# Linear attention feeding two feed-forward stages: where the queries' feature maxima are computed and how they reach the feature map

## The chip, the cores and the metric

The kernel runs on one core of one Trainium2 chip. The metric is device microseconds from the first to the last instruction of a run of the whole program. TensorE (PE in the profile), VectorE (DVE), ScalarE (ACT), GpSimd (POOL) and SyncE (SP, which only issues DMAs here) run side by side and wait for each other through semaphores; each works through its own instructions in program order.

## The reference, cut to what matters

B = H = 8, S = 576 tokens, D = 64, 128 projected features.

```python
def phi(x):                                  # q and k: (8, 8, 576, 64)
    proj = x @ w_phi                         # (..., 576, 128)
    proj = proj - max(abs(proj), axis=-1)    # one maximum per token and head
    return concatenate([exp(proj), exp(-proj)], axis=-1)
q_p, k_p = phi(q), phi(k)
kv  = k_p^T @ v;  z = sum_s k_p
att = (q_p @ kv) / (q_p @ z + 1e-6)          # -> x, (8, 576, 512)
# first feed-forward (phase 1): token shift, xk, xr
y = sigmoid(xr @ w_r) * (relu(xk @ w_k)**2 @ w_v)
# second feed-forward (phase 2)
h = relu(y @ w_in); out = (h * sigmoid(conv3(h))) @ w_out
```

## The kernel before, in words

The program has two phases. Phase 2 (the second feed-forward) isn't touched. Phase 1 does, for each of the 8 batches, the attention of four pairs of heads and the first feed-forward ("MoE" below). It is software-pipelined: one iteration does the MoE of batch m and the attention of batch m+1. `batches` (L338) makes it a prologue (attention of batch 0 alone, with the split of the ten weight pieces in it), an unrolled iteration, a loop of six, and a last iteration with MoE only.

The order of work inside an iteration is written by a planner. `attention_steps` (L48) lists the steps of the four pairs; `iteration` (L81) walks through them with estimated TensorE durations (`PE_NS`, L38) and after a step puts in as many MoE tiles as `FILL_NS` (L41) says, so that TensorE has work while VectorE and ScalarE prepare the next step. The same list of steps drives all engines, so an engine never does a later step's work before an earlier one's. A tile is 12 matmuls of 288 columns in fp32r (each product done in three parts, high and low halves): K tiles (`tile_k`, L558) are drained on ScalarE by relu, square and square again (L678, L681, L683) and one VectorE subtract (L818); R tiles by one tanh (L699); V tiles, two units long, by one VectorE instruction (L825). One iteration has 16 K, 8 R and 16 V units: 480 matmuls.

A pair's steps before the change, with TensorE's instructions (an fp32 matmul shows as two):

- QP: project the queries token by token (tokens on partitions), 10 matmuls of 128 columns, in the two 64-row halves of the array (`project`, L481). VectorE takes the largest magnitude per token from PSUM (L756) and splits it in two fp32r parts (L761, L763).
- KP: the same for the keys, into the same banks, so it waits for L756. VectorE takes the maxima (L767) and subtracts them (L771).
- M: five transposes turn the maxima into rows (L503); ScalarE copies them to SBUF (L644).
- EK: ScalarE makes exp of the shifted keys and of their negative (L649, L651).
- P0, P1: for each half of the tokens, project the queries again with features on partitions (two matmuls of 288 columns) and subtract the maxima by a matmul with a matrix `pick` of -1 rows (two more), all in 64-row halves (`feature_rows`, L507). ScalarE then makes the exponentials (L657).
- KV: sum over tokens, 20 matmuls of 65 columns (`sum_kv`, L522), and a copy (L663).
- DEN, NUM: denominators and numerators (`sum_den` L534, `attend` L548), 8 matmuls of 288 columns each, in 32-column and 64-column quarters and halves of the array; two copies (L668, L673).
- RC, DV: the denominators go to 64 partitions by DMA (L383), VectorE inverts them (L777, L780), they go through DRAM and back (L388, L392), and VectorE divides (L785). Then follow the token shift and its splits (XK/HK/LK and XR/HR/LR, L797, L805, L694, L813).

In PSUM the attention has three banks (ps0) and two (ps1), the MoE three (psm). In the prologue odd pairs use psm instead of ps0, so that a pair's projections can run ahead of the one before.

Of the kernel before, what the change touches and what calls it, by code (L numbers as in the profile page):

```python
# [11 lines left out]
P = 128  # L12
# [6 lines left out]
TT = 5  # L19
# [6 lines left out]
ROWS = D + 2  # L26
# [21 lines left out]
def attention_steps():  # L48

    steps = [("QP", 0)]  # L50
    for p in range(PAIRS):
        steps += [(s, p) for s in ("KP", "M", "EK", "P0", "KV", "P1", "DEN", "NUM")]
        steps += [("QP", p + 1)] if p + 1 < PAIRS else []
    return steps


def first_attention_steps():

    steps = [("QP", 0), ("KP", 0)]
    for p in range(PAIRS):  # L60
        last = p == PAIRS - 1

        def ahead(s):
            return [(s, 0, "next") if last else (s, p + 1)]
# [16 lines left out]
def iteration(with_moe, with_next, ran_ahead=False):  # L81
# [38 lines left out]
    if with_next:  # L120
        fill(FIRST_FILL)
        for step in attention_steps():
            s, p = step[:2]
            if not (ran_ahead and step in (("QP", 0), ("KP", 0))):
                emit(step)
            if with_moe:
                fill(FILL_NS.get(s, 0))
                if s == "DEN":
                    later += [(now + RC_AFTER, ("RC", p)), (now + DV_AFTER, ("DV", p))]
                    later.sort(key=lambda t: t[0])  # L130
                if (s, p) == ("DEN", PAIRS - 1):
                    fill(LAST_FILL)
# [62 lines left out]
def phase_1(nc, ctx, q, k, v, w_phi, mu_k, mu_r, w_k, w_v, w_r, y_scr, den_scr, w_in):  # L195
# [18 lines left out]
    pick = sb_att("pick", [P, F], F32R)  # L214
# [3 lines left out]
    q_max, k_max = sb_att("q_max", [P, 2, TT]), sb_att("k_max", [P, 2, TT])  # L218
    q_max_split = sb_att("q_max_split", [P, TT, 2, D], F32R)
    max_rows = sb_att("max_rows", [P, TT * P], F32R)  # L220
# [3 lines left out]
    pick_f = k_exp[:, 0, 0, :]  # L224
# [19 lines left out]
    ps1 = ctx.enter_context(nc.psum_tensor("ps1", [P, 2 * BANK], F32))  # L244
# [5 lines left out]
    rows_zeroed, tail_zeroed, banks_zeroed, x_zeroed = sem("rows_zeroed"), sem("tail_zeroed"), sem("banks_zeroed"), sem("x_zeroed")  # L250
# [5 lines left out]
    q_projected, k_projected, shared_bank = sem("q_projected"), sem("k_projected"), sem("shared_bank")  # L256
    q_max_ready, q_max_hi, q_max_split_ready = sem("q_max_ready"), sem("q_max_hi"), sem("q_max_split_ready")
    k_max_ready, k_shifted = sem("k_max_ready"), sem("k_shifted")
    max_turned, max_rows_ready = sem("max_turned"), sem("max_rows_ready")
# [3 lines left out]
    den_summed, den_copied = sem("den_summed"), sem("den_copied")  # L263
# [26 lines left out]

    def att_psum(p, a):
        return psm[:].rearrange("p b s -> p (b s)") if first_of(a) and p % 2 == 1 else ps0[:]

    def await_att_psum(eng, p, a):

        if first_of(a):
            await_(eng, den_copied, PAIRS, a, p - 1)
        elif second_of(a) and p == 0:
            eng.wait_ge(den_copied, PAIRS - 1)
        else:  # L300
            await_(eng, den_copied, PAIRS, a, p)
# [19 lines left out]
    def await_bank(eng, t, batch):  # L321
# [3 lines left out]
        if before < 0 and first_of(batch):  # L325
            eng.wait_ge(den_copied, PAIRS)
# [11 lines left out]
    def batches(eng, work):  # L338

        work(None, (None, 0), first_attention_steps())  # L340
        work((None, 0), (None, 1), iteration(True, True, ran_ahead=True))
# [3 lines left out]

    def attention_of(step, a):

        return (None, 1) if step[-1] == "next" else a
# [4 lines left out]
    def _(sp):  # L353

        def load_qk(p, a):

            reg, off = a
            await_(sp, features, H, a, 2 * (p - 1))
# [35 lines left out]
        def work(m, a, steps):  # L394
            if a is not None and not second_of(a):
# [12 lines left out]
            if a is not None and second_of(a):  # L408
                load_qk(1, a)
            pieces = 2  # L410
            for step in steps:
                kind = step[0]
                of = attention_of(step, a)
                if kind == "QP" and step[1] + 1 < PAIRS and step[-1] != "next":
                    load_qk(step[1] + 1, a)
                elif kind == "QP" and step == ("QP", PAIRS - 1) and m is None:
                    load_qk(0, (None, 1))
                if kind == "KV" and step[1] + 1 < PAIRS:
                    load_v(step[1] + 1, a)
                if m is None and kind in ("QP", "KP", "P1") and pieces < len(PIECES):  # L420
# [16 lines left out]
                if kind == "DEN":  # L437
                    spread_den(step[1], of)
                if kind == "RC":
                    repeat_den(step[1], of)  # L440
# [12 lines left out]
    def _(pool):  # L453
        nc.gpsimd.memset(v_nat[:], 0.0).then_inc(zeroed, 1)
        nc.gpsimd.memset(ident[:], 0.0).then_inc(ident_ready, 1)
        nc.gpsimd.memset(pick_f, 0.0).then_inc(pick_made, 1)
# [3 lines left out]
        for n, row in enumerate((0, 1, D, D + 1)):  # L460
            pool.wait_ge(pick_made, 1 + n)
            nc.gpsimd.affine_select(out=pick_f, in_=pick_f, compare_op=ALU.not_equal, fill=-1.0,
                                    base=-row, pattern=[[0, F]], channel_multiplier=1).then_inc(pick_made, 1)
# [693 lines left out]
```

## Time and profile before

| | |
|---|---|
| median of 3 runs | 1418.75 us (1409.08 to 1427.29) |
| the profiled execution | 1417.62 us |
| its span (first to last instruction) | 1415.8 us |
| TensorE busy | 1360.0 us, 96% |
| VectorE, ScalarE busy | 672.6 us (48%), 626.6 us (44%) |
| mean granted TensorE clock | 0.984 of full speed |
| phase 1 ends about | 987 us |

The span is the time from the first to the last instruction of the profiled execution, 1.8 us less than its own time. The busy times of the engines overlap. A matmul's end in the trace is modelled and reaches past the start of the next, so the distance from start to start is what a matmul costs in a stream.

### The profile page before, as it was taken

The numbers are of one execution on the slowest core, as the hardware profiler recorded it, in microseconds if no ns is written. First come the engines' busy times: TensorE is split into PE (matmuls) and PEld (weight loads), VectorE is DVE, ScalarE is ACT, GpSimd is POOL, SyncE is SP. The second block draws the span as 40 slices with busy tenths as digits, with TensorE's granted clock in tenths as the row PEclk, the third lists the DMA queues.
The fourth block names the chain that finished last, engine by engine and source line by source line (L and its number), as shares of the span: only waits on it lengthen the run. The fifth ranks groups of instructions, "written<-read, shape, count | busy, mean of one in ns | idle before, by whom it ended". The sixth has DMA issues, their size and how long they took to land. (4 is left out here: it accounts for less than half of the span.)

```text
span 1415.8 us, 26326 instructions
## 1 busy us (share of the span) xinstructions
PE 1360.0 (96%) x10368; PEld 1211.6 (86%) x10368; DVE 672.6 (48%) x1047; ACT 626.6 (44%) x1111; POOL 13.5 (1%) x18
## 2 busy tenths in 40 slices
PE   5879999999999999999999999998899999999998
PEld 4668899889888889888988888998788988998997
DVE  5444244334433624442544362451757556655753
ACT  3536345454352534545445353443444443433532
POOL 0000000000000000000000000000300000000000
PEclk9879999999999999999999999999999999999999
DMA  5411202202212120220221212030310210110101
GB/s 165 124 45 40 58 27 77 63 20 69 61 45 70 40 58 26 62 78 19 70 54 53 69 41 58 25 116 22 93 64 1 71 64 30 41 63 30 41 30 38
DMA packets 94579, 78.60 MB, mean 56 GB/s; under 512 B 64656, under 2 KB 72976, under 8 KB 93456
## 3 DMA queue, kind: packets, MB, share of 16 engines
q1 hardware_dynamic: 94480, 77.10, 18.2%
q8 instruction: 84, 1.38, 0.4%
q14 instruction: 15, 0.12, 0.0%
HBM read 57.75 MB, written 19.02 MB: 54 GB/s over the span
## 5 line engine op out<-in xcount | busy, mean ns | idle before, releaser
L472 PE MATMUL psm<-xk_hi,wk_hi 128*128 128x288 f32 x512 | 158.6, 310 | 15.1 <-issue 6.9
L969 PE MATMUL psh<-y_hi,win_hi 128*128 128x288 f32 x512 | 153.9, 301 | 13.4 <-ACT h L1054 9.0
L818 DVE TENSOR_TENSOR k_lo<-square,k_hi 128x288 fp32r<-128x288 f32 x128 | 58.7, 458 | 221.3 <-ACT square L683 221.3
L472 PE MATMUL psm<-k_hi,wv_hi 128*128 128x288 f32 x512 | 154.4, 302 | 0.0
L472 PE MATMUL psm<-xk_lo,wk_hi 128*128 128x288 f32 x512 | 153.7, 300 | 0.0
L472 PE MATMUL psm<-xk_hi,wk_lo 128*128 128x288 f32 x512 | 153.2, 299 | 0.0
L970 PE MATMUL psh<-y_lo,win_hi 128*128 128x288 f32 x512 | 152.2, 297 | 0.0
L971 PE MATMUL psh<-y_hi,win_lo 128*128 128x288 f32 x512 | 151.6, 296 | 0.0
L472 PE MATMUL psm<-k_lo,wv_hi 128*128 128x288 f32 x512 | 151.1, 295 | 0.0
L472 PE MATMUL psm<-k_hi,wv_lo 128*128 128x288 f32 x512 | 150.8, 295 | 0.0
L1112 DVE SCALAR_TENSOR_TENSOR conv<-h,taps,conv 128x576 f32<-128x576 f32 x64 | 55.2, 863 | 141.3 <-ACT conv L1056 141.3
L472 PEld LDWEIGHTS psm<-xk_hi,wk_hi 128*128 128x128 f32 x512 | 98.8, 193 | 24.3 <-issue 16.3
L969 PEld LDWEIGHTS psh<-y_hi,win_hi 128*128 128x128 f32 x512 | 97.2, 190 | 16.2 <-ACT h L1054 11.3
L472 PE MATMUL ps<-q_exp,kvz 128*64 128x288 f32 (+1 forms) x992 | 102.1, 409 | 0.5 <-ACT q_exp L657 0.5
L472 PEld LDWEIGHTS psm<-k_hi,wv_hi 128*128 128x128 f32 x512 | 96.3, 188 | 6.6 <-issue 5.8
L678 ACT ACTIVATE relu<-psm 128x288 f32<-128x288 f32 x128 | 51.7, 404 | 113.4 <-PE psm L472 113.4
L971 PE MATMUL pso<-wout_hi,g_lo 128*128 128x512 f32 x256 | 101.1, 395 | 0.0
L969 PE MATMUL pso<-wout_hi,g_hi 128*128 128x512 f32 x256 | 101.0, 395 | 0.0
L970 PE MATMUL pso<-wout_lo,g_hi 128*128 128x512 f32 x256 | 101.0, 394 | 0.0
L1054 ACT ACTIVATE h<-psh 128x576 f32<-128x576 f32 x64 | 41.8, 653 | 129.4 <-DVE gated L1100 94.3
L472 PEld LDWEIGHTS psm<-xk_hi,wk_lo 128*128 128x128 f32 x512 | 98.9, 193 | 0.0
L472 PEld LDWEIGHTS psm<-xk_lo,wk_hi 128*128 128x128 f32 x512 | 98.8, 193 | 0.0
(116 smaller groups left out, 2810.9 us busy)
## 6 DMA issues: line engine op xcount, KB each, us to landing
v_nat<-in_v SPq DMA_DIRECT2D x32, 320.0 KB, 3.6
qk<-in_q SPq DMA_DIRECT2D x32, 288.0 KB, 2.9
qk<-in_k SPq DMA_DIRECT2D x32, 288.0 KB, 3.2
den<-den_scr SPq DMA_DIRECT2D x64, 144.0 KB, 3.0
y_scr<-y SPq DMA_DIRECT2D x64, 144.0 KB, 1.8
y<-y_scr SPq DMA_DIRECT2D x8, 1152.0 KB, 5.5
out<-rows SPq DMA_DIRECT2D x32, 256.0 KB, 2.0
den_parts<-den_rows SPq DMA_DIRECT2D x128, 2.2 KB, 1.9
```

Source lines behind the costliest of these rows:

```text
L472: return nc.tensor.matmul(o, lhsT, rhs, start=first, stop=last)
L678: nc.scalar.activation(relu[:, i % 2, :], psm[:, UNIT["K", n, i] % 3, 0:HALF], ACT.Relu).then_inc(k_relu, 1)
L818: nc.vector.tensor_tensor(k2_lo[:, i, :], square[:, i % 2, :], k2_hi[:, i, :].bitcast(F32), ALU.subtract).then_inc(k2_lo_ready, 1)
L969: nc.tensor.matmul(o, wh, xh, start=first, stop=False, skip_group_check=True)
L970: nc.tensor.matmul(o, wh, xl, start=False, stop=False, skip_group_check=True)
L971: return nc.tensor.matmul(o, wl, xh, start=False, stop=last, skip_group_check=True)
L1054: nc.scalar.activation(two(h[:, j % 2, 1:1 + S]), psh[:, j % 2, :, 0:HALF], ACT.Relu, scale=0.5).then_inc(h_ready, 1)
L1112: nc.vector.scalar_tensor_tensor(out=conv[:, j % 2, :], in0=h[:, j % 2, 0:S], scalar=taps[:, 0, j:j + 1], in1=conv[:, j % 2, :], op0=ALU.m ...
```

## The change

A pair's steps become E, M, KS, PICK, EK, KV, DEN, NUM:

- E (`features_and_keys`): one projection of the queries, features on partitions, left raw in ps0 (four matmuls of 512, 512, 64 and 64 columns), and the ten key tiles of 128 columns, eight into ps1 and two into ps0; all in 64-row halves. It waits for the numerators' copy of the pair before, and three times for matmuls of its own.
- VectorE, `part_maxima`: two transposes in blocks of 32 x 32 of the raw features (576 columns each, from PSUM), maxima and subtract for the last key tile of each head, a reduce of the 1152 turned columns to 36, a copy.
- M: one 128-column transpose. VectorE, `spread_maxima`: a reduce of 128 columns, the split in two parts (32 columns each), and a multiply by a 0/1 mask that spreads the maxima into 18 blocks of 32 columns.
- KS (`shift_keys`): maxima and subtract for the other eight key tiles (1024 columns each).
- PICK (`subtract_maxima`): four matmuls with `pick`, now on all 128 rows, 512 and 64 columns for each head, added onto the raw features. ScalarE makes four exponentials of 576 columns.
- DEN and NUM have the same columns, cut in 64 and 512 instead of twice 288. Both copies follow NUM.
- The copy L644, four of the five transposes, the ten token-by-token query projections, and the prologue's second PSUM home for the next batch's first pair (QP and KP "next") are gone.

The core of the diff:

```diff
-PE_NS = {"QP": 1100, "KP": 1100, "M": 550, "P0": 800, "P1": 800, "KV": 2240, "DEN": 1000, "NUM": 1950,
+PE_NS = {"E": 2800, "M": 150, "PICK": 700, "KV": 4500, "DEN": 1200, "NUM": 2200,
-FILL_NS = {"QP": 2200, "M": 1600, "P0": 3500, "P1": 2600}
-FIRST_FILL, LAST_FILL, RC_AFTER, DV_AFTER = 6000, 1600, 3500, 9000
+FILL_NS = {"E": 3200, "M": 1600, "PICK": 4800, "KV": 1600, "NUM": 1600}
+FIRST_FILL, RC_AFTER, DV_AFTER = 3000, 3800, 9500
...
-    steps = [("QP", 0)]
-        steps += [(s, p) for s in ("KP", "M", "EK", "P0", "KV", "P1", "DEN", "NUM")]
-        steps += [("QP", p + 1)] if p + 1 < PAIRS else []
+    return [(s, p) for p in range(PAIRS) for s in ("E", "M", "KS", "PICK", "EK", "KV", "DEN", "NUM")]
...
-        steps += [("M", p)] + before("RC") + [("P0", p), ("EK", p)] + ahead("QP")
-        steps += [("KV", p), ("P1", p)] + before("DV") + ahead("KP") + [("DEN", p), ("NUM", p)]
+        steps += [("M", p), ("KS", p)] + before("RC") + [("EK", p), ("PICK", p), ("KV", p)] + before("DV")
+        steps += [] if last else [("E", p + 1)]
+        steps += [("DEN", p), ("NUM", p)]
...
+        def features_and_keys(p, a):
...
+            key_tile(0, TT - 1).then_inc(shared_bank, 1)
+            feature_chunk(1, 1, True)
+            feature_chunk(0, 0, True)
+            await_(pe, shared_bank, 3 * PAIRS, a, 3 * p + 1)
+            key_tile(1, TT - 1).then_inc(shared_bank, 1)
+            key_tile(0, 0)
+            key_tile(1, 0)
+            await_(pe, shared_bank, 3 * PAIRS, a, 3 * p + 2)
+            feature_chunk(0, 1, True).then_inc(shared_bank, 1)
+            key_tile(1, 1)
+            key_tile(0, 1)
+            await_(pe, shared_bank, 3 * PAIRS, a, 3 * p + 3)
+            feature_chunk(1, 0, False).then_inc(raw_features, 1)
+            for t in range(2, TT - 1):
+                for h in range(2):
+                    last = key_tile(h, t)
...
+        def part_maxima(p, a):
+            await_(dve, raw_features, PAIRS, a, p + 1)
+            for h in range(2):
+                nc.vector.transpose(q_turn[:, h, :], q_cols(h, p, a)).then_inc(q_turned, 1)
+            nc.vector.tensor_reduce(k_max[:, :, TT - 1], k_tail(p, a), AX.X, ALU.max, apply_absolute_value=True).then_inc(k_tail_max, 1)
...
+            nc.vector.tensor_reduce(q_part[:].rearrange("p (h c) -> p h c", h=4)[:, 0:2, 0:TOK],
+                                    q_turn[:].rearrange("p h (j f) -> p h j f", f=32), AX.X, ALU.max,
+                                    apply_absolute_value=True).then_inc(q_part_once, 1)
...
+        def spread_maxima(p, a):
+            await_(dve, max_turned, PAIRS, a, p + 1)
...
+            nc.vector.tensor_tensor(max_blocks[:], own_block[:].unsqueeze(2).to_broadcast([P, TOK, 32]),
+                                    q_max_split[:].bitcast(F32).unsqueeze(1).to_broadcast([P, TOK, 32]), ALU.mult).then_inc(blocks_ready, 1)
```

The planner's fills give, for one iteration, this order around the waits of the changed steps (K+ is a short third part of a K tile, V- the first half of a V tile): E0, K+ x3, K3, M0, K4, KS0, PICK0, K5, K6, K7, EK0, KV0; E1, R2, RC0, R3, XR, M1, V-0, KS1, PICK1, V0, V-1, V1, EK1, KV1; E2, V-3, RC1, V3, M2, K0, K1, KS2, PICK2, K2, K3, K4, EK2, KV2; E3, K7, RC2, R0, M3, R1, KS3, PICK3, R2, R3, V-0, EK3, KV3.

## Rows read from the trace of the kernel before

**Rows 1.** the page: TensorE's busy time, and its granted clock in 40 slices
```profile
PE 1360.0 (96%) x10368; PEld 1211.6 (86%) x10368; DVE 672.6 (48%) x1047; ACT 626.6 (44%) x1111; POOL 13.5 (1%) x18
...
PEclk9879999999999999999999999999999999999999
```

**Rows 2.** busy time in one loop iteration; columns PE, PEld, DVE, ACT, POOL, clock, DMA
```profile
332.40:450.00 117.60, 116.55 (x996) 102.99 (x996) 49.62 (x84) 54.83 (x104) 0.00 (x0) 1.00 0.19 53
```

**Rows 3.** timeline of TensorE: start us, length, engine, line; steps of one pair
```profile
293.25 1.39 PE L472 MATMUL ps<-phi,qk 64*128 64x128 f32 x20
...
294.57 0.74 PE L503 MATMUL ps<-ident,q_max_split 128*66 128x128 f32 x5
...
295.06 0.38 PE L472 MATMUL psm<-xk_hi,wk_hi 128*128 128x288 f32 x1
...
302.51 2.34 PE L472 MATMUL ps<-v_nat,k_exp 128*128 128x65 f32 x20
...
307.01 0.76 PE L472 MATMUL ps<-qk,phi 64*128 64x288 f32 x4
...
307.83 0.40 PE L472 MATMUL psm<-xr_hi,wr_hi 128*128 128x288 f32 x1
...
309.61 1.15 PE L472 MATMUL ps<-q_exp,kvz 128*1 128x288 f32 x16
...
310.69 0.40 PE L472 MATMUL psm<-xr_hi,wr_hi 128*128 128x288 f32 x1
...
312.48 2.16 PE L472 MATMUL ps<-q_exp,kvz 128*64 128x288 f32 x16
```

**Rows 4.** timeline of TensorE inside a tile of the MoE half
```profile
300.26 0.30 PE L472 MATMUL psm<-xk_lo,wk_hi 128*128 128x288 f32 x1
300.39 0.29 PE L472 MATMUL psm<-xk_hi,wk_lo 128*128 128x288 f32 x1
```

**Rows 5.** timeline of ScalarE at the same place
```profile
301.85 0.41 ACT L678 ACTIVATE relu<-psm 128x288 f32<-128x288 f32 x1
...
302.98 0.39 ACT L678 ACTIVATE relu<-psm 128x288 f32<-128x288 f32 x1
...
304.08 0.39 ACT L678 ACTIVATE relu<-psm 128x288 f32<-128x288 f32 x1
...
304.85 0.43 ACT L683 ACTIVATE square<-relu 128x288 f32<-128x288 f32 x1
```

**Rows 6.** costliest groups, ScalarE and VectorE: busy us, mean ns of one | idle before
```profile
L657 ACT ACTIVATE q_exp<-ps 128x576 f32<-128x576 f32 x128 | 75.6, 642 | 17.5 <-PE ps L472 17.5
...
L805 DVE SCALAR_TENSOR_TENSOR mix<-diff,mu,x 128x288 f32<-128x288 f32 x128 | 60.0, 511 | 2.8
...
L771 DVE TENSOR_TENSOR k_shift<-ps,k_max 128x1280 f32<-128x1280 f32 x30 | 44.7, 1491 | 1.0
...
L767 DVE TENSOR_REDUCE k_max<-ps 128x10 f32<-128x1280 f32 x30 | 44.2, 1475 | 18.1 <-PE ps L472 18.1
...
L649 ACT ACTIVATE k_exp<-k_shift 128x1280 f32<-128x1280 f32 x32 | 40.7, 1271 | 12.9 <-DVE k_shift L771 12.6
...
L785 DVE TENSOR_TENSOR x<-num,den 128x576 f32<-128x576 f32 x32 | 24.1, 754 | 7.0 <-DMA den<-den_scr 7.0
```

**Rows 7.** timeline of SyncE's queue and VectorE, a denominator's round trip
```profile
311.59 2.39 SPq L383 DMA_DIRECT2D den_parts<-den_rows  x4
...
315.36 0.17 DVE L777 SCALAR_TENSOR_TENSOR den_cols<-den_parts 128x9 f32<-128x9 f32 x1 [9.59 <-DMA den_parts<-den_rows]
...
317.24 1.11 SPq L392 DMA_DIRECT2D den<-den_scr  x2
```

**Rows 8.** timeline of TensorE at the end of a loop iteration
```profile
451.05 0.37 PE L472 MATMUL psm<-xk_hi,wk_hi 128*128 128x288 f32 x1 [2.10 <-issue]
```

**Rows 9.** busy time shortly after it, columns as in rows 2
```profile
452.00:455.30 3.30, 3.30 (x16) 3.30 (x15) 0.00 (x0) 0.00 (x0) 0.00 (x0) 0.50 0.80 249
```

**Rows 10.** timeline of TensorE, first matmul of the MoE half
```profile
94.37 0.58 PE L472 MATMUL psm<-xk_hi,wk_hi 128*128 128x288 f32 x1 [4.46 <-DVE xk_lo L813]
```

More of the change, by code:

```diff
@@ L123, in iteration @@
             s, p = step[:2]
-            if not (ran_ahead and step in (("QP", 0), ("KP", 0))):
-                emit(step)
+            emit(step)
             if with_moe:
                 fill(FILL_NS.get(s, 0))
-                if s == "DEN":
+                if s == "NUM":
                     later += [(now + RC_AFTER, ("RC", p)), (now + DV_AFTER, ("DV", p))]
                     later.sort(key=lambda t: t[0])
-                if (s, p) == ("DEN", PAIRS - 1):
-                    fill(LAST_FILL)
         if with_moe:
@@ L394, in work @@
         def work(m, a, steps):
-            if a is not None and not second_of(a):
+            if a is not None:
                 load_qk(0, a)
@@ L436, in work @@
                         sp.dma_start(early.y[:], y_scr[0]).then_inc(early.y_loaded, 16)
-                if kind == "DEN":
-                    spread_den(step[1], of)
+                if kind == "NUM":
+                    spread_den(step[1], a)
                 if kind == "RC":
-                    repeat_den(step[1], of)
+                    repeat_den(step[1], a)
                 if kind == "V":
@@ L459, in _ @@
                                 pattern=[[-1, P]], channel_multiplier=1).then_inc(ident_ready, 1)
[L460 to L463, printed above, removed]
+        nc.gpsimd.memset(own_block[:], 0.0).then_inc(own_made, 1)
+        for q in range(4):
+            pool.wait_ge(own_made, 1 + q)
+            nc.gpsimd.affine_select(out=own_block[:], in_=own_block[:], compare_op=ALU.not_equal, fill=1.0, base=-32 * q,
+                                    pattern=[[-1, TOK]], channel_multiplier=1).then_inc(own_made, 1)
         pool.wait_ge(zeroed, 1)
@@ L471, in mm @@
         def mm(o, lhsT, rhs, first, last):
-            return nc.tensor.matmul(o, lhsT, rhs, start=first, stop=last)
+            return nc.tensor.matmul(o, lhsT, rhs, start=first, stop=last, skip_group_check=True)
         def three(o, w_parts, x_parts, first, last):
@@ new lines, in turn_maxima, with subtract_maxima @@
+        def turn_maxima(p, a):
+            await_(pe, q_part_ready, PAIRS, a, p + 1)
+            nc.tensor.matmul(turned_max(p, a), q_part[:], ident[:], start=False, stop=True, is_transpose=True,
+                             skip_group_check=True).then_inc(max_turned, 1)
+        def subtract_maxima(p, a):
+            await_(pe, blocks_ready, PAIRS, a, p + 1)
+            for h in range(2):
+                for chunk in CHUNKS[h]:
+                    cols = slice(*chunk)
+                    last = mm(q_cols(h, p, a)[:, cols], pick[:, h, :], max_blocks[:].rearrange("q j t -> q (j t)")[:, cols], False, True)
@@ L536, in sum_den @@
             await_(pe, kvz_copied, PAIRS, a, p + 1)
-            await_(pe, q_exp_ready, 2 * H, a, 4 * p + 4)
-            ps = att_psum(p, a)
-            for n in range(2):
-                cols = slice(HALF * n, HALF * n + HALF)
+            await_(pe, q_exp_ready, 4 * PAIRS, a, 4 * p + 4)
+            for chunk in CHUNKS[1]:
+                cols = slice(*chunk)
                 for h in range(2):
@@ L758, in max_q @@
+        def spread_maxima(p, a):
+            await_(dve, max_turned, PAIRS, a, p + 1)
+            nc.vector.tensor_reduce(q_max[:], turned_max(p, a).rearrange("q (i t) -> q t i", i=4), AX.X, ALU.max).then_inc(q_max_ready, 1)
             await_(dve, q_max_ready, PAIRS, a, p + 1)
-            await_(dve, max_turned, PAIRS, a, p)
-            hi, lo = (q_max_split[:, :, :, part].rearrange("p t h -> p h t") for part in range(2))
-            nc.vector.tensor_copy(hi, q_max[:]).then_inc(q_max_hi, 1)
+            nc.vector.tensor_copy(q_max_split[:], q_max[:]).then_inc(q_max_hi, 1)
+            low = slice(P // 2, P)
```

256 lines of the change are left out of this document (114 added, 142 removed).

## The prediction

> **What bounds the kernel now.** I read the page first [rows 1]: TensorE is busy 96% of the span, VectorE and ScalarE under half, and the clock is full from the fourth slice on. Then one loop iteration [rows 2]: 116.55 of 117.60 us busy, 996 matmul records; with the gap at its end [rows 8] it lasts 118.65. In the timeline of TensorE no step of the attention waits inside the loop: the MoE tiles that the planner puts between the steps cover what ScalarE and VectorE do. So in the loop the kernel pays for TensorE's work alone, and two questions decide: how much TensorE work goes, and whether the new chain of helpers is still covered.
>
> The work in one iteration: a MoE matmul costs 0.131 us from start to start [rows 4], 480 of them 63.1. The rest of 116.55, 53.4 us, is four pairs, 13.35 each. By steps [rows 3]: KP 293.25 to 294.57 = 1.32 (QP is the same twenty instructions), M 0.49, KV 302.51 to 307.01 = 4.50, P1 307.01 to 307.83 = 0.82 (P0 the same), DEN 1.08, NUM about 2.1. These add up to 12.4. The other 0.9 stands in the tiles beside them: the 12 matmuls between DEN and NUM take 1.79 (310.69 to 312.48 [rows 3]) instead of 12 x 0.131 = 1.57. Going from the full array to a split one or back costs some 0.2 us, half of it on each side. A pair has ten such changes (around KP, P0, P1, QP, DEN and NUM).
>
> **The change, part by part, on TensorE.**
> - Goes: QP's and KP's columns (1.11 each without their change, 1.32 less 0.2), M 0.49, P0 and P1 0.62 each, and five array changes, 1.0 (PICK and the new M use the full array, as KV and MoE do). Together 4.95.
> - E comes. Ten key tiles are five in each half of the array, two instructions of 0.111 each (KP's 1.11 by 10 [rows 3]), so 1.11 per half. The 576 feature columns of a head are two instructions of 512 at some 0.43 (DEN's 288 columns: 0.97/4 = 0.242) and two of 64, bounded by 0.05 and 0.11: about 1.05. With 0.2 for the waits on its own matmuls and the unlike sizes side by side: 2.4. Bounds 2.2 (the halves fully side by side) and 3.3 (no gain from the halves in the large chunks).
> - M 0.11. PICK: 512 columns at the MoE rate are 0.22, twice, and two small ones under 0.1: 0.6. DEN and NUM each have a small round besides the large: +0.05 to +0.1 each, 0.15.
> - Sum: 2.4 + 0.11 + 0.6 + 0.15 = 3.3 against 4.95: 1.65 less per pair (0.7 to 1.9), 6.6 per iteration.
>
> On E a rule speaks against me. DEN's 16 instructions of 0.242 take 0.97 net [rows 3], so four quarters work at once although each matmul is two instructions. The Trainium skill, "TensorE: Matmul & The Clock Gate", Part 3, says that matmuls start strictly in program order. By that rule a 512-column matmul's second pass would hold up the other half: E would be about 2.85, 0.45 more per pair, some 12 us over the run. The trace of DEN doesn't fit it.
>
> **On the helpers, where the stalls come from.** An engine follows the one list of steps.
>
> VectorE after E (from the raw features, 2.15 us into E): two transposes of 576 columns from PSUM. The reduce of 1280 gives 1.15 ns a column (L767 [rows 6]), so 0.66; the 576-column multiply takes 0.75 (L785 [rows 6]); I take 0.72 each (bounds 0.6 and 1.5, no row shows one). Two tail operations of 256 columns at 0.35, the reduce of 1152 at 1.35, a copy 0.2: 3.7, and 0.1 for semaphores. Then M, then `spread_maxima`: 0.3 + 0.4 + 0.8 = 1.5. Then KS: two of 1024 columns, 2.5 by L767 and L771 [rows 6]. In all 7.8 us a pair where two thirds of that did before; VectorE has the room on average, not at these places:
> - M waits for the first chain. The fill is two units, 3.16, plus the last 0.45 of E: 0.15 short for pairs 1 to 3. For pair 0 the fill is 2.8, and the chain starts behind the last mixes of the batch before: numerators done, denominators copied out 1.0 later (0.35 and 0.65, a 576-column ScalarE copy priced as L657 [rows 6]), the round trip 3.8 + 0.4 + 1.4 + 3.5 [rows 7], another 2 behind other VectorE work, DV and the two short mixes 4.7: 17 us, just when E0's features are there. 0.8 short. Together 1.2.
> - PICK waits for the second chain, 0.35 + 1.5 after M, against one unit of fill (two for pair 2). In pair 0 VectorE must first make the low half of K3, and ScalarE has a backlog there: K0 to K3 end within 2.8 us and take it 1.1 each (301.85 to 302.98 to 304.08 [rows 5]). 2.4 short. In pair 1 the three-instruction mix of XR, 1.4 (L805 three times [rows 6]), stands in front: 1.7. In pair 3 K7's low half: 0.7. Together 4.8.
> - KV waits for exp(keys). EK stands behind the whole fill of PICK in the list, so ScalarE does four exponentials of the queries (0.56 each from start to start), then the drains of K5, K6, K7, and only then EK. K7 ends where KV wants to start; its drain takes 0.2 + 1.1 and L649 1.27 [rows 6]: at least 2.6 short, I take 2.7 for pair 0, 3.0 for pair 2 (same three K tiles, some backlog), 0.4 for pair 3, nothing for pair 1 (V tiles, which ScalarE doesn't drain). Together 6.1. The kernel before shows the price: its KV at 302.51 [rows 3] follows three K tiles too, and ScalarE drains them until 305.28 [rows 5]; it doesn't wait because EK stood ahead of them. In the new order that place would wait 2.8 + 1.3 = 4.1.
>
> Stalls: 1.2 + 4.8 + 6.1 = 12.1 a loop iteration, between 6 (KV's 2.6 twice and little else) and 19 (transposes of 1.5). Net +5.5; seven iterations have attention (the unrolled one and six): +38.5. The copy L644 that ScalarE saves is not on these chains. E waits for both copies of the NUM before it: 0.35 + 1.3 against a unit of fill and an array change, 1.8, so nothing, and if that cover went, 0.1 to 0.3 each. Behind E's waits only TensorE's own tiles queue. E0's loads are issued at the iteration's start, 3.6 ahead of E0, and land about when it wants them; a late load shows as E0's wait instead of M0's, since VectorE is busy until then. SyncE's queue has the same DMAs in nearly the same order, with `den_parts` after NUM instead of DEN, which only DV sees.
>
> **The prologue.** Before, MoE starts at 94.4 [rows 10]. Now a pair's chain is: E to `spread_maxima` 6.3, from there spread, a weight piece (1024 columns, 1.2 by L771), KS, both EKs, the second half of KV, its copy: 11.9; and on the next pair VectorE does a third weight piece after both copies of NUM, ahead of its `spread_maxima`, which makes 6.3 into 9.6. First spread at 14, then 21.5 a pair, and after the fourth some 18 to the first xk: 14 + 64.5 + 18.5 = 97. +3, bounds -6 and +12.
>
> **The clock.** After the one 2.10 us gap at a loop's end the clock reads 0.50 for 3.3 us, 16 matmuls where some 25 would fit [rows 8, 9]: 1.7 us lost on the stretch. The other loop ends have shorter gaps and no fall. Now each iteration would have three gaps of 2.4 to 3.0. I take two falls, of which one half is absorbed where the next stall is another engine's: 1.5 x 1.7 x 7 = 18. Bounds 0 and 45.
>
> Sum against the profiled execution's own 1417.6 (the median of the runs shown is 1.1 higher): + 38.5 + 3 + 18 = 1477; as a median 1478. A difference under about 2% can't be told from none here.
>
> **Rivals.**
> - *The work removed wins (faster).* All stalls are covered, because transposes and small operations are cheap and the backlogs smaller: 1.65 x 28 pairs = 46 less, with a prologue as before 1372. For it: VectorE is only half busy and the fills after E and PICK are the longest. Against: EK's place in the list, which no duration mends. It decides if the stalls of an iteration stay under 6.6; KV0 and KV2 alone need 5.2. Chance 0.11.
> - *Even.* The two KV stalls and a little at PICK, 6 to 8 an iteration, no clock falls: net within 1.5 an iteration, 1410 to 1435. Chance 0.17.
> - *Stalls, but the clock holds.* The gaps are each short and TensorE stays at 2.4 GHz: 1417.6 + 41 = 1459. It is inside my range; 0.25, slower over 2%.
> - *Clock falls after every large stall*, three or more an iteration, E at 2.85 or slow transposes (+3 at each M and PICK): 1510 to 1530. 0.12.
> - *My forecast*, 1478 give or take 15: 0.35.
>
> Slower by over 2% (above 1447) 0.72, within 2% 0.17, faster 0.11. Eight in ten: 1422 to 1525; both lower cases would be reached only in part.
>
> **What would show it.** Right: the waits of TensorE have M, PICK and KV by VectorE's copy, the mask multiply and L649's successor; KV0 and KV2 wait 2.6 to 3 each and all E 2.4 to 2.9 long; an iteration of 122 to 127 us without its end gap; more slices of PEclk under 9; TensorE's busy time lower although the span is longer. Wrong: no wait at KV (then EK isn't where I read it), iterations under 114, transposes far from 0.72, or a first MoE matmul outside 88 to 106.

## The result and the profile after: 11% slower

| | before | after |
|---|---|---|
| median | 1423.02 us (4 runs, 1409.08 to 1428.69) | 1583.67 us (4 runs, 1578.22 to 1588.85) |
| ratio | | 1.1145 (95%: 1.1049 to 1.1240) |
| span of the profiled execution | 1415.8 us | 1583.9 us |
| mean granted clock | 0.984 | 0.908 |
| first MoE matmul | 94.37 | 119.97 |
| first MoE matmul to the start of phase 2 | 897.4 us | 1037.8 us |
| phase 2 | 424.1 us | 426.1 us |

Slower was the forecast, but 1583.67 lies 58.67 above the upper end of my range. Of the 168.1 us between the two spans, 25.6 came in the prologue, 140.4 in the pipelined part and 2.0 in phase 2.

The page of the kernel after: busy time of TensorE, then its granted clock in 40 slices (before: [rows 1]).

```profile
PE 1428.9 (90%) x9600; PEld 1271.0 (80%) x9600; DVE 753.5 (48%) x1275; ACT 598.9 (38%) x1079; POOL 13.1 (1%) x18
...
PEclk7567989889798988989998998989989999999999
```

There are 768 matmuls fewer and yet 68.9 us more of busy time. The clock row says why: over half of the slices of phase 1 (15 of 29) read 8 or less, where before only two of the whole row did, both in the prologue. Matmuls ran at 1.2 GHz for part of the time. Next, a loop iteration of the kernel after in the timeline of TensorE (start, length, what runs, idle time before it and its releaser; the steps that waited, and what stands behind two of them):

```profile
397.57 0.37 PE L462 MATMUL psm<-xk_hi,wk_hi 128*128 128x288 f32 x1 [2.14 <-issue]
...
405.25 0.34 PE L462 MATMUL ps<-phi,qk 64*128 64x128 f32 x1 [2.34 <-DMA qk<-in_k]
...
412.54 0.33 PE L508 MATMUL ps<-ident,q_part 128*128 128x128 f32 x1
...
416.67 0.95 PE L462 MATMUL ps<-max_blocks,pick 128*128 128x512 f32 x4 [2.20 <-DVE max_blocks L766]
...
424.85 3.17 PE L462 MATMUL ps<-v_nat,k_exp 128*128 128x65 f32 x20 [2.47 <-ACT k_exp L634]
427.82 4.47 PE L462 MATMUL ps<-v_nat,k_shift 128*128 128x65 f32 x20
432.05 0.59 PE L462 MATMUL psm<-xr_hi,wr_hi 128*128 128x288 f32 x1
432.43 0.44 PE L462 MATMUL psm<-xr_lo,wr_hi 128*128 128x288 f32 x1
...
484.45 4.53 PE L462 MATMUL ps<-v_nat,k_exp 128*128 128x65 f32 x20 [2.50 <-ACT k_exp L634]
488.78 4.47 PE L462 MATMUL ps<-v_nat,k_shift 128*128 128x65 f32 x20
```

To be seen: the waits stand where the prediction put them. PICK0 waits 2.20 for the mask multiply, KV0 2.47 and KV2 2.50 for exp of the keys. PICK1 waits 1.07 (450.08). M0 doesn't wait: E0 had waited 2.34 for its keys. In the next iteration E0 waits 4.15, and the other four are 2.21, 2.47, 1.07 and 2.50. The two iterations have 11.9 and 14.1 us of idle time. Without their end gaps, 1.29 and 1.74, which the forecast counted apart, that is 10.6 and 12.4, and I had forecast 12.1. The second thing to see is KV's length. KV2 takes 4.33 for its first half (484.45 to 488.78) where it takes 2.18 at full clock (179.66 to 181.84), and the MoE matmuls at 432.43 are 0.24 apart instead of 0.131 [rows 4]. Busy time and clock (next to last but one column) in windows of the kernel after, columns as in [rows 2]:

```profile
397.57:536.63 139.06, 126.86 (x900) 111.76 (x901) 58.84 (x113) 51.23 (x100) 0.00 (x0) 0.89 0.17 45
...
424.90:426.30 1.40, 1.40 (x13) 1.40 (x14) 1.28 (x4) 1.20 (x1) 0.00 (x0) 1.00 0.05 12
...
426.50:436.60 10.10, 10.10 (x56) 8.74 (x55) 0.99 (x3) 0.80 (x2) 0.00 (x0) 0.50 0.14 32
484.50:498.00 13.50, 13.50 (x68) 11.70 (x68) 0.46 (x1) 2.77 (x5) 0.00 (x0) 0.50 0.11 24
436.60:484.40 47.80, 44.28 (x350) 38.63 (x346) 25.01 (x47) 19.91 (x38) 0.00 (x0) 1.00 0.21 58
```

So after a wait of 2.5 us at KV the clock is at 0.50 for 10 to 14 us, where [rows 9] show 3.3. That holds for 11 of the 14 such waits of the trace; behind the other three (704.12, 762.13 and 898.35) it was 6.8. Over the trace, stretches at 0.50 ("half-clock time" below) add up as follows:

| half-clock us | before | after |
|---|---|---|
| prologue, up to the first MoE matmul | 24.7 | 82.7 |
| pipelined part, from there to phase 2 | 13.3 | 194.7 |
| phase 2 | 9.7 | 15.2 |
| sum | 47.7 | 292.6 |

Work in them takes twice as long, so where TensorE is always at work, half of the difference is time lost. In the pipelined part that is (194.7 - 13.3) / 2 = 91 of the 140.4 us. For the whole run it would be 122, but in the prologue TensorE also waits inside these stretches, so there the half is an upper bound. One loop iteration went from 118.65 to 139.7 (mean of these two, the longest; the next two take 134.4 and 136.4), +21.1: the clock 30.7 / 2 = 15.4, idle time 13.0 - 2.1 = 10.9, less some 4 to 5 of work that is gone. The first MoE matmul stands in the timeline of the kernel after (before: [rows 10]):

```profile
119.97 0.58 PE L462 MATMUL psm<-xk_hi,wk_hi 128*128 128x288 f32 x1 [3.29 <-DVE xk_lo L815]
```

The groups of VectorE's new operations, kernel after (busy us, mean ns of one | idle before):

```profile
L742 DVE STREAM_TRANSPOSE q_turn<-ps 128x576 f32<-128x576 f32 x60 | 43.4, 762 | 40.2 <-PE ps L462 40.2
L750 DVE TENSOR_REDUCE q_part<-q_turn 128x36 f32<-128x1152 f32 x32 | 43.0, 1343 | 0.0
...
L766 DVE TENSOR_TENSOR max_blocks<-own_block,q_max_split 128x576 fp32r<-128x576 f32 x32 | 24.3, 759 | 1.4 <-DVE q_max_split L763 0.3
```

I had priced them at 0.72, 1.35 and 0.8. ScalarE ahead of KV0, kernel after (timeline): four exponentials of the queries, the drains of K5, K6 and K7, and only then L634 for the keys, which KV0 at 424.85 waits for.

```profile
417.74 2.28 ACT L643 ACTIVATE q_exp<-ps 128x576 f32<-128x576 f32 x4 [1.94 <-PE ps L462]
...
422.42 0.41 ACT L663 ACTIVATE relu<-psm 128x288 f32<-128x288 f32 x1 [0.18 <-PE psm L462]
...
423.55 1.25 ACT L634 ACTIVATE k_exp<-k_shift 128x1280 f32<-128x1280 f32 x1
```

### The profile page after: what moved, and what is told of

It is laid out like the page before. It is cut to its first block and busy times, and to the rows that moved or that the text cites. A ratio compares the mean times of both kernels' runs of the same rounds, so it can differ in the third digit from the quotient of the medians.

```text
span 1583.9 us, 24972 instructions
## 1 busy us (share of the span) xinstructions
PE 1428.9 (90%) x9600; PEld 1271.0 (80%) x9600; DVE 753.5 (48%) x1275; ACT 598.9 (38%) x1079; POOL 13.1 (1%) x18
## 5 line engine op out<-in xcount | busy, mean ns | idle before, releaser
L462 PE MATMUL psm<-xk_hi,wk_lo 128*128 128x288 f32 x512 | 158.7, 310 | 0.0
L462 PE MATMUL ps<-v_nat,k_exp 128*128 128x65 f32 x640 | 102.5, 330 | 48.9 <-ACT k_exp L634 48.5
L462 PEld LDWEIGHTS ps<-v_nat,k_exp 128*128 128x128 f32 x640 | 98.3, 243 | 55.7 <-ACT k_exp L634 34.5
L827 DVE SCALAR_TENSOR_TENSOR y<-gate,psm 128x288 f32<-128x288 f32 x64 | 28.9, 451 | 199.0 <-PE psm L462 199.0
L462 PEld LDWEIGHTS psm<-xk_hi,wk_hi 128*128 128x128 f32 x512 | 104.3, 204 | 18.7 <-issue 12.9
L462 PEld LDWEIGHTS ps<-phi,qk 64*128 64x128 f32 x632 | 84.1, 218 | 37.5 <-DMA qk<-in_q 17.3
L462 PE MATMUL ps<-v_nat,k_shift 128*128 128x65 f32 x640 | 113.8, 355 | 0.0
L462 PEld LDWEIGHTS ps<-v_nat,k_shift 128*128 128x128 f32 x640 | 111.1, 271 | 0.0
L462 PE MATMUL ps<-phi,qk 64*128 64x128 f32 x632 | 82.8, 319 | 28.1 <-DMA qk<-in_k 21.0
L462 PEld LDWEIGHTS psm<-xk_lo,wk_hi 128*128 128x128 f32 x512 | 104.1, 203 | 0.6
```

The costliest lines, as they stand in the source:

```text
L462: return nc.tensor.matmul(o, lhsT, rhs, start=first, stop=last, skip_group_check=True)
L827: nc.vector.scalar_tensor_tensor(out=y[:, i % 2, :], in0=gate[:, i, :], scalar=1.0, in1=psm[:, UNIT["V", n, i] % 3, 0:HALF], op0=ALU.add, ...
```

## The experiments

Theory: the chain of waits is as forecast, and the surplus over the forecast of some 100 us is TensorE at 1.2 GHz after each wait at KV. Rivals: the new work itself costs more than I priced, or the clock falls because KV's and E's matmuls are sparse, waits or not. e1 to e4 shared one chip and its runs of the kernel before (median 1418.04 us); beside e5 to e7 that kernel took 1423.72, beside e8 and e9 1420.13, beside e10 and e11 1421.96. e1 to e7 have two runs each. The intervals of e4 and e5 overlap that of e1, and the interval of e7 overlaps that of the kernel after; for these three the medians decide little, and what is said rests on the traces. In e2, e5 and e7 to e11 extra matmuls are added whose results nobody reads.

**e1: EK directly behind PICK, ahead of the MoE tiles that follow it.** Only ScalarE's order changes.

```diff
-FILL_NS = {"E": 3200, "M": 1600, "PICK": 4800, "KV": 1600, "NUM": 1600}
+FILL_NS = {"E": 3200, "M": 1600, "EK": 4800, "KV": 1600, "NUM": 1600}
```

> The changed kernel with EK (both exponentials of the keys) ahead of PICK's fill of MoE tiles instead of behind it; nothing else moves. Clock theory: the two 2.5 us waits of KV0 and KV2 in each iteration go, and with them the half-clock stretches of 10 and 13.5 us that begin there (in the changed kernel's trace 426.5 to 436.6 and 484.5 to 498), worth another 10 to 12 us an iteration; KV runs in 4.5 us throughout; 1584 falls by 85 to 120 us to 1465 to 1500. Rival (the waits cost only themselves, the rest of the loss lies in E, the transposes and the new order): 7 x 5 = 35 us less, about 1549.

Measured 1476.06 us, 1.0378 of before (1.0242 to 1.0514): 107.6 less than the kernel after. Hardly any wait at KV in the loop (0.2 at most), half-clock time 121.8, of it 44.5 in the pipelined part. TensorE's page row and the clock, then a whole iteration, of e1:

```profile
PE 1358.4 (92%) x9600; PEld 1210.9 (82%) x9600; DVE 754.2 (51%) x1275; ACT 598.4 (41%) x1079; POOL 13.7 (1%) x18
...
PEclk9658999999999999999999999999999999999999
```

```profile
366.23:486.28 120.05, 113.71 (x900) 100.83 (x901) 59.30 (x113) 51.37 (x100) 0.00 (x0) 0.99 0.18 52
```

The same 9600 matmuls have 70.5 us less of busy time. The pipelined part fell from 1037.8 to 925.1 us, by 112.7. The KV waits of seven iterations are 7 x 4.97 = 35 of it, and the clock (194.7 - 44.5) / 2 = 75: together 110. The prologue, whose order is the same, has 62.0 us of half-clock time instead of 82.7, and still its first MoE matmul came at 122.42 and not sooner than 119.97. What e1's trace lacks is the fall over the first pair, where TensorE often waits; there it cost nothing.

**e2: 17 matmuls of 288 columns into a free bank, ahead of KV0 and KV2.** They fill the wait with work.

```diff
         def sum_kv(p, a):
             await_(pe, v_loaded, 16 * PAIRS, a, 16 * (p + 1))
+            if not first_of(a) and p in (0, 2):
+                await_(pe, k_shifted, PAIRS, a, p + 1)
+                for _ in range(17):
+                    mm(ps1[:, 1, 0:HALF], wk_hi[:, 0, 0:P], wk_hi[:, 0, 0:HALF], True, True)
```

> The changed kernel with 17 extra matmuls of 288 columns (0.131 us each, 2.2 us) into the free bank of ps1 just ahead of KV0 and KV2 in every iteration with MoE; their result is never read, the order and all waits of the rest stay. They fill the 2.5 us in which TensorE stood idle, and take away nothing. Clock theory: KV runs at the full clock, KV0 and KV2 take 4.5 instead of about 8 us, 50 to 85 us less, 1500 to 1535, although TensorE does more work. Rival (idle time alone is what costs): the same 1584, or up to 15 more.

Measured 1519.77 us, 1.0686 (1.0543 to 1.0829): 64 less than the kernel after, with 238 matmuls (31 us at 0.131) more. KV of pair 0 in e2 (timeline):

```profile
402.80 0.95 PE L462 MATMUL ps<-wk_hi 128*128 128x288 f32 x6
403.98 2.45 PE L462 MATMUL ps<-v_nat,k_exp 128*128 128x65 f32 x20 [0.23 <-ACT k_exp L638]
406.27 2.40 PE L462 MATMUL ps<-v_nat,k_shift 128*128 128x65 f32 x20
```

Both KV halves now take 2.3 each. KV starts when it did, and the work in between costs nothing, since it replaces idle time. What is won is the clock alone: half-clock time is 143.4, of it 50.9 in the pipelined part, (194.7 - 50.9) / 2 = 72 us, against 65.3 measured there (1037.8 to 972.5).

**e3: the kernel before with EK behind P0.** The same misplacement, with nothing else of the change.

```diff
-        steps += [(s, p) for s in ("KP", "M", "EK", "P0", "KV", "P1", "DEN", "NUM")]
+        steps += [(s, p) for s in ("KP", "M", "P0", "EK", "KV", "P1", "DEN", "NUM")]
```

> The kernel before, with one edit: EK behind the fill of P0 instead of ahead of it, as the changed kernel has it. Theory that EK's place makes the stall: KV0 and KV3 wait 1.9 to 4 us for exp of the keys (about 5 to 7 us an iteration) where nothing waited. Clock theory on top: the clock falls at these waits and KV stays at half of it, 4 to 5 us more for each, so 1419 becomes 1510 to 1540. Rival without the clock: 1419 + 7 x 6 = 1460. If EK's place is innocent: 1419.

Measured 1579.94 us, 1.1109 (1.0961 to 1.1256). One word moved in the list costs the kernel before 162 us, as much as the whole change. It is 40 more than the upper end of what the clock theory had asked for: three KVs of an iteration wait and not two (pairs 0, 2 and 3: 1.75, 2.56 and 2.56). Waits of TensorE by total, KV of pair 3 in the timeline, and the window behind its wait, of e3:

```profile
PE ps L472 <- ACT k_exp L649: 50.5, 23, 2.6
```

```profile
346.88 4.07 PE L472 MATMUL ps<-v_nat,k_exp 128*128 128x65 f32 x20 [2.56 <-ACT k_exp L649]
350.74 4.47 PE L472 MATMUL ps<-v_nat,k_shift 128*128 128x65 f32 x20
```

```profile
347.40:361.10 13.70, 13.70 (x67) 11.76 (x70) 0.00 (x0) 2.63 (x5) 0.00 (x0) 0.50 0.00 1
```

In the pipelined part KV waits 7 x 6.87 = 48 us, and the clock costs (222.8 - 13.3) / 2 = 105: 153 together, against 151.4 measured there (897.4 to 1048.8). For every microsecond that KV waits, TensorE loses more than two in what follows. Behind the waits of 2.56 the clock fell every time, behind those of 1.75 in four iterations of seven.

**e4: e1 with 6000 instead of 3000 ns of fill ahead of E0** (FIRST_FILL), so that E0 finds its keys loaded.

```diff
-FIRST_FILL, RC_AFTER, DV_AFTER = 3000, 3800, 9500
+FIRST_FILL, RC_AFTER, DV_AFTER = 6000, 3800, 9500
```

> As e1, and the first fill of an iteration 6.0 instead of 3.0 us, so E0 comes after four K tiles and its two loads have landed; M0 and PICK0 have VectorE free of the mixes. Both the 2.3 to 4.2 us wait of E0 for its keys and most of PICK0's 2.2 us should go: 1584 falls by what e1 gives and 25 to 55 more, to 1425 to 1465. If the loop's remaining loss is E's own length or the changed tail of the iteration, it stays within 15 of e1.

Measured 1495.07 us, 1.0512 (1.0374 to 1.0650), 19 slower than e1: a miss. Largest waits of TensorE in e4:

```profile
PE psm L462 <- DVE xk_lo L815: 40.3, 16, 5.7
PE ps L462 <- DVE max_blocks L766: 38.6, 23, 4.9
```

E0's wait is gone, but the third K tile now wants a part of x that VectorE hasn't split yet (3.79 at 386.08; the first tile waits 2.14 at 378.48), and the PICKs together wait longer (1.28, 2.02 and 1.39 for pairs 0 to 2, against 2.02 and 1.07 in e1). The half-clock time is 125.2, nearly the 121.8 of e1. So these waits, with dense MoE work (288-column matmuls) behind them, cost their own length and hardly any clock.

**e5: e1, and in the prologue 26 small matmuls behind each M and 18 behind each PICK.**

```diff
+        def idle_work(p, a, n):
+            if not first_of(a):
+                return
+            await_(pe, num_copied, PAIRS, a, p)
+            other = ps0[:] if p % 2 == 1 else psm[:].rearrange("p b s -> p (b s)")
+            for _ in range(n):
+                mm(other[:, 2 * BANK:2 * BANK + 2 * F], pick[:, 0, :], pick[:].rearrange("p h f -> p (h f)"), True, True)
```

> e1 with extra matmuls of 256 columns in the prologue alone: 26 after each M and 18 after each PICK (about 0.11 us each, 2.9 and 2.0 us), into a bank that holds nothing, never read. They stand in the 5 and 3.4 us in which TensorE waits for VectorE and ScalarE. Clock theory: the prologue's half-clock stretches (20.5 us of every 27 in e1) go or shrink, E takes 2.8 instead of 4.2 and KV 4.5 instead of 9.2 us, and the first MoE matmul comes at 100 to 105 instead of about 120: 1476 falls to 1455 to 1462. Rival (the prologue is long by its chain of waits, as I priced it, and the clock only looks on): 1476 or up to 8 more.

Measured 1467.14 us, 1.0319 (1.0209 to 1.0430): 9 less than e1, between the two expectations. The first MoE matmul starts at 106.69 instead of 122.4. The pairs of the prologue take 21.0, 21.4 and 25.4 us and not 27.3 to 27.8, and its half-clock time went from 62.0 to 27.3, of which half is 17. Of the 15.7 us won there 8.3 are lost again in the pipelined part, 5.8 of them because E0 waits longer for its keys (23.1 us in all against 17.3). So the clock accounts for about half of the prologue's 25.6: 13.3 are gone and 12.3 left. How much is gone varies: e10 has the same prologue, its trace shows 48.2 us of half-clock time there, and its first MoE matmul comes at 116.53.

**e6: e1 with the fill put ahead of PICK.**

```diff
-FILL_NS = {"E": 3200, "M": 1600, "EK": 4800, "KV": 1600, "NUM": 1600}
+FILL_NS = {"E": 3200, "KS": 3200, "EK": 3200, "KV": 1600, "NUM": 1600}
```

> e1 with the fills between maxima and PICK made two tiles instead of one (3.2 after KS, which now follows M directly) and those before KV two instead of three (3.2 after EK). PICK0 and PICK1, which wait 2.0 to 2.4 and 1.1 us in e1, should wait under 0.5 together, and KV still nothing, if the chain of spread_maxima is what they wait for: 7 x 3 = 21 us less and a fall of the clock fewer here and there, 1440 to 1455. If ScalarE's four exponentials of the queries and two of the keys (4.9 us against 3.8 of cover) now come too late, KV waits 1 us or more again, the clock falls with it, and it is slower than e1.

Measured 1516.30 us, 1.0665 (1.0552 to 1.0778), 40 slower than e1. PICK0 waits 0.42 only, but KV1 now waits 2.30. ScalarE in e6 ahead of it (timeline), and TensorE's window behind it:

```profile
425.94 0.45 ACT L679 ACTIVATE xr_hi<-mix 128x288 fp32r<-128x288 f32 x1 [3.33 <-DVE mix L807]
426.29 2.25 ACT L643 ACTIVATE q_exp<-ps 128x576 f32<-128x576 f32 x4
428.41 1.29 ACT L634 ACTIVATE k_exp<-k_shift 128x1280 f32<-128x1280 f32 x1
```

```profile
431.00:441.00 10.00, 10.00 (x55) 9.50 (x58) 0.00 (x0) 0.39 (x2) 0.00 (x0) 0.50 0.15 33
```

ScalarE stood 3.33 us for a mix that VectorE had behind KS. A wait of 2.30 at another pair's KV brings the same 10 us at half the clock. In the pipelined part, 44 us longer than in e1, the half-clock time grew by 68.0, half of which is 34; KV's waits grew by 27 (13.5 to 40.5) and PICK's fell by 19 (30.3 to 10.9).

**e7: e2's 17 matmuls behind the wait instead of ahead of it.** The wait stays, then comes dense work, then KV.

```diff
+                if not first_of(a) and p in (0, 2) and e == 0:
+                    for _ in range(17):
+                        mm(ps1[:, 1, 0:HALF], wk_hi[:, 0, 0:P], wk_hi[:, 0, 0:HALF], True, True)
```

> The changed kernel with the 17 extra matmuls of e2 behind the wait for exp of the keys instead of ahead of it: TensorE still stands idle for 2.5 us before KV0 and KV2, then does 2.2 us of dense work, then KV. If the idle time by itself brings the clock down, it falls as in the changed kernel (10 to 14 us at half from there) and the 14 fillings come on top, 4 us or more each at half clock: 1584 becomes 1620 to 1650. If it is the idle time together with KV's sparse work behind it, the dense matmuls hold the clock and KV runs in 4.5 us: 1584 + 31 - 70 = 1530 to 1560.

Measured 1569.11 us, 1.1037 (1.0919 to 1.1154): 15 less than the kernel after although it does 31 us more work and waits as long. It lies between the two expectations. Timeline and windows of e7:

```profile
419.50 4.05 PE L462 MATMUL ps<-wk_hi 128*128 128x288 f32 x17 [2.47 <-ACT k_exp L637]
423.35 2.38 PE L462 MATMUL ps<-v_nat,k_exp 128*128 128x65 f32 x20
425.56 2.40 PE L462 MATMUL ps<-v_nat,k_shift 128*128 128x65 f32 x20
```

```profile
420.00:423.30 3.30, 3.30 (x16) 3.30 (x15) 2.13 (x5) 0.75 (x1) 0.00 (x0) 0.50 0.00 0
423.50:436.00 12.50, 12.50 (x111) 9.98 (x109) 1.06 (x2) 3.43 (x7) 0.00 (x0) 1.00 0.13 28
```

The same idle 2.47 still starts the fall, but it lasts 3.4 us instead of 10 to 14, and KV runs at full clock. So idle time brings the clock down, and what comes next decides how long it stays: with KV's 40 matmuls of 65 columns it stays down, with 288-column matmuls it is back soon. KV's work alone does not lower it, as e1 and e2 show. What it is in KV that keeps the clock down, the width of its matmuls, their weight loads or their being fp32, no run tells apart.

**e8: the best of these together.** e5, plus: pair 0's fill split around KS and EK, pair 1's mix XR behind M1, and the next batch's first q and k loaded at E3 of the iteration before (the loop's last iteration is unrolled for that).

```diff
+                early_pick = {"KS": 3200, "EK": 3200} if p == 0 else {"M": 1600}
+                fill(early_pick.get(s, FILL_NS.get(s, 0)))
...
+            out.insert(j, out.pop(i))
...
+                elif kind == "E" and not (a[0] is None and a[1] == LAST):
+                    load_qk(0, (a[0], a[1] + 1))
```

> The changed kernel with every wait that the runs so far named taken on: EK ahead of the fill (e1), the prologue's extra matmuls (e5), for pair 0 KS directly behind M and two tiles before and after PICK (e6's cure for PICK0, without its wait at KV1), XR's three-instruction mix behind the spread of pair 1, and the next batch's first q and k loaded three pairs ahead (for that the last loop iteration is unrolled). If waits and clock are all that the changed kernel loses, an iteration falls from 121.7 (e1) to about 114 and the run to 1400 to 1425, and TensorE's saved work (1.2 us a pair in these runs) first shows. If moving the waits only makes new ones, as in e6, it stays at 1445 or above.

Measured 1434.97 us, 1.0106 (1.0049 to 1.0163): a miss, though 149 us below the kernel after. One iteration of it:

```profile
343.04:461.61 118.57, 114.05 (x900) 100.91 (x901) 59.16 (x113) 51.37 (x100) 0.00 (x0) 0.99 0.18 53
```

118.57 is what the kernel before takes with its end gap [rows 2, 8]. The waits left are 1.4 to 2.0 at the iteration's start, 1.96 at M0 and 0.43 each at PICK0 and KV0 (in three other iterations 0.77 at KV0 and none at PICK0). What the change takes off TensorE is spent on them. The pipelined part takes 897.8 us against 897.4 before; what e8 is slower by is its prologue, 106.73 against 94.37.

**e9 and e11: the kernel before with dense matmuls in its prologue** (60 in each of four places, then 32 and 30), in case what helped e5 helps it too.

```diff
+            for _ in range(n):
+                mm(att_psum(p, (None, 0))[:, 0:F], pick[:], pick[:], True, True)
...
+                idle_work(p - 1, 60)
```

> The kernel before, with 60 extra matmuls of 128 columns (about 0.06 us each) ahead of M of pairs 1 to 3 and behind the last NUM of the prologue, where TensorE idles for 3.8 to 4.5 us; never read. The clock reads half for 34 us of its prologue. Clock theory: most of these stretches go, and where TensorE sets the pace there (75 to 94 us) time falls: 3 to 9 us less in all. If its prologue is set by the weight pieces and SyncE's queue, nothing or up to 2 us more.

> e9 with about half the extra matmuls (32 ahead of each M, 30 behind the last NUM); e9 showed 0.11 us each, so 3.5 us where TensorE idles 3.8 to 4.5, instead of 6.8. Clock theory: the prologue's half-clock time shrinks as in e9 (34 to 27 us or less) without e9's overlong filling, 1420 becomes 1412 to 1420. If the prologue is set by pieces and queue: 1420 to 1424.

Measured 1432.36 us, 1.0093 (1.0063 to 1.0123), and 1426.48 us, 1.0049 (1.0023 to 1.0075): misses both. The 60 matmuls take 6.8 us (28.10 to 34.86 in the timeline of e9), longer than the idle time they were to fill, and the first MoE matmul comes at 110.18. With 32 it stands at 96.95 and nothing is won. Half-clock time in the prologue hardly went down, from 24.7 to 23.9 and 17.1, so whether the clock holds up this prologue isn't shown by these two.

**e10: e8 with the tile behind KV0 moved ahead of M0.**

```diff
-                early_pick = {"KS": 3200, "EK": 3200} if p == 0 else {"M": 1600}
+                early_pick = {"E": 4800, "KS": 3200, "EK": 3200, "KV": 0} if p == 0 else {"M": 1600}
```

> e8 with pair 0's tile between KV and DEN moved to between E and M. In e8 M0 waits 2.0 us for part_maxima, and the clock falls there in most iterations (3.4 us at half). Expected: M0 waits under 0.5, DEN0 now waits 0.5 to 0.7 for the copy of KV, the clock holds: 1.4 + 1.7 us less an iteration, 1435 becomes 1412 to 1425, as fast as the kernel before or a little faster. If VectorE's late start at E0 only pushes the wait on to PICK0 or KV0, it stays at 1430 to 1440.

Measured 1435.97 us, 1.0086 (1.0057 to 1.0114): the first expectation is missed, and the second, that the wait only moves on, came true. Its iteration, with no clock fall in it:

```profile
352.78:472.02 119.24, 112.91 (x901) 99.45 (x901) 59.93 (x113) 51.32 (x100) 0.00 (x0) 1.00 0.19 52
```

M0's wait shrank to 0.48 and PICK0's grew to 1.54. The chain over VectorE is as long as it was, and moving a tile moves the wait. No version beat the kernel before.

The accounts together, for the pipelined part of the profiled executions, where TensorE sets the pace. The difference in half-clock time, halved, stands beside the difference in waits at KV and the measured difference:

| from, to | half-clock us | halved | KV's waits | measured |
|---|---|---|---|---|
| before, after | 13.3, 194.7 | +91 | +35 | +140 (other waits, and work that is gone) |
| before, e3 | 13.3, 222.8 | +105 | +48 | +151 |
| after, e1 | 194.7, 44.5 | -75 | -35 | -113 |
| after, e2 | 194.7, 50.9 | -72 | filled, -32 | -65 (31 of work added) |
| after, e7 | 194.7, 82.3 | -56 | 0 | -17 (31 of work added) |
| e1, e4 | 44.5, 52.3 | +4 | 0 | +22 (waits for x and at PICK) |
| e1, e6 | 44.5, 112.5 | +34 | +27 | +44 (PICK's waits -19) |

## Why the prediction was wrong in size

- **The failed step is "The clock".** I took the one fall that the kernel before shows in its loop, 1.7 us lost behind a gap with dense MoE work after it [rows 8, 9], and priced every fall at that: 18 us, bound 45. In [rows 8, 9] the gap is followed by 0.131 us matmuls. The new gaps are followed by KV, and there a fall lasts mostly 10 to 14 us and costs 5 to 7 (three of fourteen last 6.8 and cost 3.4). Measured in a loop iteration: 30.7 us at half clock, 15.4 lost, and over the pipelined part 91 more than before where the sum had 18. I had also taken one of two falls as half absorbed by the next wait. The sums leave no room for that: 105 and 48 of waits in e3 against 151 measured, 75 and 35 in e1 against 113. The rival "clock falls after every large stall" had the mechanism but the same price, hence 1530.
- **A longer fall stood in the trace of the kernel before, in its prologue.** KV of pair 3 waits 1.42 there (after two shorter waits of 0.84 and 0.79), and then the clock is at 0.50 for 10.1 us, all of them busy:

```profile
75.35 3.48 PE L472 MATMUL psm<-v_nat,k_exp 128*128 128x65 f32 x20 [1.42 <-ACT k_exp L649]
78.63 4.47 PE L472 MATMUL psm<-v_nat,k_shift 128*128 128x65 f32 x20
```

```profile
76.60:86.70 10.10, 10.10 (x61) 9.47 (x64) 0.76 (x1) 1.58 (x3) 0.00 (x0) 0.50 0.04 14
```

- A rule that I had not weighed points the same way. The Trainium skill, "TensorE: Matmul & The Clock Gate", in "A second HAM failure mode: psum-queue depth-cycling", tells of a kernel whose many short pauses between groups of matmuls are enough to make the clock swing, so that its throughput suffers though its single matmuls look right. The traces agree: e3 has such pauses, of 1.75 and 2.56 us, and 222.8 us at half clock in its pipelined part. Here the matmuls behind a pause do look slow, as KV's 4.47 against 2.40 shows.
- **EK behind PICK's fill: right.** KV0 2.47 and KV2 2.50 against 2.7 and 3.0, KV1 nothing, cause and engine as told; e1 removes them by the order alone, e3 makes them in the other kernel.
- **PICK and M: partly right.** PICK0 2.20 against 2.4, PICK1 1.07 against 1.7, PICK3 nothing against 0.7. M0 hardly waits (0.42 at most in the loop), since **E0's load** is late by 1.9 to 4.2, which I had written off as "about when it wants them". Idle time without the end gaps came to 10.6 and 12.4 per iteration against 12.1: the sum is right partly by luck.
- **TensorE's work: gain too large.** I had 6.6 less per iteration. An iteration without a clock fall (e10) is busy 112.91 against 116.55, so 3.6; e1 gives 4.5 (113.71 with 1.7 of clock). E is the largest part of this: in a stretch at full clock it takes 2.78, not 2.4 (kernel after, first and last rows of an E and the MoE matmul behind it):

```profile
164.97 0.37 PE L462 MATMUL ps<-phi,qk 64*128 64x128 f32 x1
164.98 0.69 PE L462 MATMUL ps<-qk,phi 64*128 64x512 f32 x1
...
167.11 0.71 PE L462 MATMUL ps<-phi,qk 64*128 64x128 f32 x7
167.75 0.40 PE L462 MATMUL psm<-xr_hi,wr_hi 128*128 128x288 f32 x1
```

  The rule of the Trainium skill that I had set aside ("TensorE: Matmul & The Clock Gate", Part 3: matmuls start in program order) gave about 2.85, and E's own time lies nearer to that; no run here separates it from longer waits of E on its own matmuls. PICK took 0.79 (416.67 to 417.46) against 0.6.
- **A sign I gave was wrong.** I had expected TensorE's busy time to be lower; it is 68.9 higher, since the same matmuls take longer at half clock.
- **VectorE's prices: right** (762, 1343, 759 ns against 720, 1350, 800).
- **Prologue: wrong**, 119.97 against 97, outside my bounds. The chain was priced at full clock. In it four stretches of 20.5 us run at 0.50, KV takes some 8.8 instead of 4.4 (75.07 to 84.36 with 0.52 of waiting), and e5, which keeps TensorE busy there, starts the MoE half at 106.7.
- **"The work removed wins" and "even"** fell with KV's waits. Even without them (e8, e10) the iteration is level with the old one, so the change's gain on TensorE is used up by its longer VectorE chain.

Open: why waits of about the same length at PICK0 bring a fall of 3.4 us in some iterations and none in others (in e1 2.40 at 504.36 has one, 2.31 at 142.87 none), and why in e3 the wait of 1.75 at KV0 is followed by 10.2 us at 0.50 in four iterations and by none in three. e10's prologue took longer than e8's, with the same work in it (116.5 against 106.7 to the first MoE matmul). The clock accounts for that, 48.2 us at 0.50 against 27.3, halved 10.4; why it stayed down longer is open too.

## What to carry to other kernels

A wait on TensorE must be priced with what follows it: 2.5 us ahead of dense matmuls cost 2.5 to 4.2 here, ahead of 40 small ones 5.9 to 9.4, mostly over 7.5. When a list drives all engines, look at what each helper engine has queued ahead of the result that TensorE wants next: here moving EK in front of the fill, one key in a dictionary, was worth 108 us. Where a wait can't be removed, dense work in it or directly behind it, ahead of the sparse steps, is worth trying: in it (e2) it won 64 us, behind it (e7) it shortened the falls, and the 15 us won there are within the noise; both used work that nobody needs. Halve the half-clock time of a trace to see how much of a slowdown is the clock, but only in a part where TensorE sets the pace.

## What the runs showed that I had not expected

- The clock falls behind idle gaps as short as 1.75 us (e3, KV0, then 10.2 us at 0.50 in four iterations of seven), and how long it stays at 1.2 GHz depends on the work behind: 3.4 us with 288-column matmuls (e7), 7 to 14 with KV's 65-column ones, through the MoE tile and the DEN that follow.
- Adding work saves time: e2's 238 unused matmuls made the program 64 us faster.
- A VectorE transpose of 576 columns in blocks of 32 x 32, from PSUM, takes 762 ns, as much as an elementwise operation on as many columns (759).
- 60 matmuls of 128 columns on the full array take 6.8 us at full clock (e9), 0.11 each, little less than one of 288 columns at 0.131: columns alone don't set the pace there.
